# Two chained feed-forward layers behind a convolution: products that fill pauses, three slots in another order, and steps of the start moved

## The reference

```
w   = softmax(weight, axis=-1)                      # 8 heads x 7 taps
att = causal convolution of x over 7 tokens, one set of taps per head    # (4, 4096, 192)
h1  = att.reshape(16384, 192) @ w_in1               # 192 -> 2048
y1  = (h1 * cos(h1)) @ w_out1                       # 2048 -> 192
h2  = y1 @ w_in2
out = (h2 * clip(h2 + 3, 0, 6) / 6) @ w_out2
```

## Time and profile before

| | |
|---|---|
| median of 3 runs | 2235.25 us |
| the profiled execution | 2235.39 us, its span 2233.6 us |
| PE, DVE, ACT, POOL busy | 100%, 82%, 78%, 68% of the span |
| TensorE clock granted, mean | 0.999 |

### The profile page before, as it was taken

The page is one execution under the profiler, slowest core; times in us unless marked ns, Lnnn a source line. Parts: engine busy times, 40 slices in busy tenths (PEclk is TensorE's granted clock), DMA queues, the critical chain, the costliest instruction groups (busy, mean ns, idle before and its releaser), DMA issues.

```text
span 2233.6 us, 56658 instructions
## 1 busy us (share of the span) xinstructions
PE 2224.0 (100%) x19491; PEld 2200.1 (98%) x19491; DVE 1823.6 (82%) x2505; ACT 1732.6 (78%) x2841; POOL 1514.7 (68%) x1071
## 2 busy tenths in 40 slices
PE   9999999999999999999999999999999999999999
PEld 6899999999999999999999999999999999999998
DVE  8978888888888888888888888888888888888754
ACT  7888777787777877778877788777787777877775
POOL 7976666666666666766666666666666666666665
PEclk9999999999999999999999999999999999999999
DMA  4200000000000000000000000000000000000001
GB/s 107 58 8 16 15 10 4 14 14 14 14 0 14 14 14 14 0 14 14 14 14 7 7 14 14 14 13 1 14 14 14 14 0 14 14 14 7 4 6 23
DMA packets 208636, 33.27 MB, mean 15 GB/s; under 512 B 203152, under 2 KB 207248, under 8 KB 208592
## 3 DMA queue, kind: packets, MB, share of 16 engines
q1 hardware_dynamic: 205424, 32.27, 8.2%
q10 hardware_dynamic: 3168, 0.39, 0.1%
HBM read 19.92 MB, written 12.58 MB: 15 GB/s over the span
## 4 chain that ended last, share of the span: by engine, by line
PE 98%; DVE 1%; ACT 0%; DMA 0%; SPq 0%; issue 0%; DVEq 0%
PE h_ps L475 47%; PE acc L482 31%; PE acc_tail L489 21%; DVE acc L1002 0%; DMA x_in<-in_x 0%; DVE gate L930 0%; ACT pre L754 0%; DVE pre L919 0%; DVE wtail_hi L1044 0%; ACT pre L744 0%; ACT g_hi L758 0%; SPq L433 0%; ACT in_hi L887 0%; DVE acc L1001 0%; DVE xT L967 0%
## 5 line engine op out<-in xcount | busy, mean ns | idle before, releaser
L1186 POOL TENSOR_TENSOR g_lo<-gate,g_hi 128x512 fp32r<-128x512 f32 x1024 | 1470.5, 1458 | 702.1 <-ACT g_hi L758 701.2
L482 PE MATMUL acc<-g_hi,wout 64*128 64x512 f32 x4096 | 1416.4, 386 | 0.0
L475 PE MATMUL h_ps<-in_hi,win_hi 64*128 64x512 f32 x2048 | 790.7, 387 | 1.7 <-ACT in_hi L887 1.3
L489 PE MATMUL acc_tail<-g_lo,wout 64*128 64x512 f32 x2048 | 791.0, 386 | 0.0
L475 PE MATMUL h_ps<-in_lo,win_hi 64*128 64x512 f32 x2048 | 790.9, 387 | 0.0
L489 PE MATMUL acc_tail<-g_hi,wout 64*128 64x512 f32 x2048 | 790.7, 386 | 0.0
L482 PE MATMUL acc<-g_lo,wout 64*128 64x512 f32 x2048 | 790.4, 386 | 0.0
L475 PE MATMUL h_ps<-in_hi,win_lo 64*128 64x512 f32 x2048 | 790.3, 387 | 0.0
L475 PE MATMUL h_ps<-in_tail,wtail_hi 64*128 64x512 f32 x2048 | 790.0, 387 | 0.3 <-DVE in_tail L1069 0.3
L482 PEld LDWEIGHTS acc<-g_hi,wout 64*128 64x128 f32 x4096 | 753.4, 184 | 2.7 <-issue 0.3
L758 ACT ACTIVATE g_hi<-gate 128x512 fp32r<-128x512 f32 x1024 | 624.1, 631 | 114.1 <-DVE gate L933 55.0
(11 more groups left out here) (121 smaller groups left out, 2371.7 us busy)
## 6 DMA issues: line engine op xcount, KB each, us to landing
out_dram<-o_blk SPq DMA_DIRECT2D x128, 64.0 KB, 1.8
x_in<-in_x SPq DMA_DIRECT2D x126, 64.0 KB, 2.2
blk_tail<-in_x SPq DMA_DIRECT2D x62, 64.0 KB, 2.2
out_dram<-blk_tail SPq DMA_DIRECT2D x62, 64.0 KB, 1.8
stage<-in_moe_w_out SPq DMA_DIRECT2D x7, 384.0 KB, 3.3
stage<-in_moe_w_in SPq DMA_DIRECT2D x3, 512.0 KB, 4.4
stage<-in_moe_w_in SPq DMA_DIRECT2D x6, 256.0 KB, 3.9
pre<-in_moe_w_in SPq DMA_DIRECT2D x2, 256.0 KB, 4.6
```

The lines of the kernel that those rows point to most:

```text
L475: return pe.matmul(chunk_of(h_ps, q, half), w, x, start=start, stop=stop)
L482: return pe.matmul(acc[pair][:, :], wout[layer][rows, 2 * q + half, cols], g[rows, :], start=start, stop=stop)
L489: return pe.matmul(acc_tail[pair][:, :], wout[layer][rows, 2 * q + half, P:2 * P], g[rows, :], start=start, stop=stop)
L1186: pool.tensor_tensor(chunk_of(g_lo, q, half), chunk_of(gate, q, half), chunk_of(g_hi, q, half).bitcast(F32), ALU.subtract).then_inc(glo_re ...
```

## The change

- PE gets five pairs of products (`bridge`) between `convolve_tails` and the first slot. Their result, written to `h_ps` of slot 1, is overwritten there.
- Slot 0's first five products are made in the order 0, 2, 3, 4, 1 (the one with `in_lo` last), and ACT and DVE split tile 0's tail ahead of its main columns.
- In slots 0 to 2 PE's UP products are placed otherwise: slot 1 completes its own at its end, and the two products of `convolve_second` stand at the ends of slots 1 and 2.
- ACT rounds weight piece 5 in slot 0 behind the cosines and rounds `g_hi` of slot 0 in slot 1; DVE rounds piece 7 in slot 2 instead of 1, and POOL makes its rest in slot 3 instead of 2. One step of tile 1's convolution moves from slot 2 to 3 and one from 3 to 4.
- The two diagonals for `convolve_second` are made by DVE, not by POOL.
- `KEEP_1` goes from 0 to 6 and `LOW_TAIL_1` from 2 to 7.

```diff
-        HIGH_BY_DVE = {0: {0: 6, 1: 7, 3: 8, 5: 9}, ...
+        HIGH_BY_DVE = {0: {0: 6, 2: 7, 3: 8, 5: 9}, ...
-        STEP_ORDER = [0, 2, 1, 3, 4]
+        STEP_ORDER, FIRST_ORDER = [0, 2, 1, 3, 4], [0, 2, 3, 4, 1]
-        CONV_FIRST = [2, 2, 3, 5, 6, 7, 7, 7, 7]
+        CONV_FIRST = [2, 2, 3, 4, 5, 7, 7, 7, 7]
-        KEEP_1, TWIN_1, TAIL_1, LOW_TAIL_1, HIGH_1, LOW_1 = 0, 1, 2, 2, 5, 6
+        KEEP_1, TWIN_1, TAIL_1, LOW_TAIL_1, HIGH_1, LOW_1 = 6, 1, 2, 7, 5, 6
...
             def rest_of_upper(i, ph, q):
 
-                if 0 < q <= LAG and i < 4:
+                if q in (1, LAG) and i < 4:
                     first_upper(5 + i, ph, q - 1, ph.base + q - 1)
-                if 0 < q <= SECOND_BY_PE and i == 4:
-                    convolve_second(q - 1)
...
+                if q == 1:
+                    for i in range(5, 9):
+                        first_upper(i, ph, q, ph.base + q)
+                if q > 0:
+                    convolve_second(q - 1)
...
+            def bridge(count):
+
+                w = win_hi[L1]
+                for _ in range(count):
+                    for rows, half in ((LOW, 0), (UP, 1)):
+                        pe.matmul(chunk_of(h_ps, 1, half), w[rows, 0:P], w[rows, 0:TOK], start=True, stop=True)
...
             convolve_tails()
+            pe.wait_ge(whi_done, 1)
+            bridge(BRIDGE_PAIRS)
             phase(first_phase())
...
+                    if ph.setup == 0 and q == 1:
+                        high_half(0, 0, 0)
...
-                    high_part(q, slot, ph.setup != 0 or q >= G_BUFS, 1 if ph.setup in (0, 1) else 2)
+                    if ph.setup == 0 and q == 0:
+                        weight_high(5)
+                    else:
+                        high_part(q, slot, ph.setup != 0 or q >= G_BUFS, 1 if ph.setup in (0, 1) else 2)
...
+            act.wait_ge(tails_convolved, 1)
+            split_tail(acc_tail[1][0:DT, :], L2)
             for half in range(2):
...
-            act.wait_ge(tails_convolved, 1)
-            split_tail(acc_tail[1][0:DT, :], L2)
-            act.wait_ge(hi_ready[L2], 2)
+            act.wait_ge(hi_ready[L2], 1)
             split_twin(in_tail[L2][0:DT, :].bitcast(F32), L2)
-            for n in (4, 5):
-                weight_high(n)
+            weight_high(4)
...
+            dve.wait_ge(eye_step, 3)
+            for t in range(SECOND_BY_PE):
+                dve.tensor_scalar(diagonal_main(t), eye, taps[:, MAIN, t:t + 1], None,
+                                  ALU.mult).then_inc(main_diag_ready, 1)
...
-            pool.wait_ge(taps_ready, QUADS)
-            for t in range(SECOND_BY_PE):
-                pool.tensor_scalar(diagonal_main(t), eye, taps[:, MAIN, t:t + 1], None, ALU.mult).then_inc(diag_ready, 1)
```

More of the change, by code:

```diff
@@ L18 @@
 WARM_PAIRS = 9
+BRIDGE_PAIRS = 5
 G_BUFS = 4
@@ L201, in conv_moe_kernel @@
         diag_ready = sem("diag_ready")
+        main_diag_ready = sem("main_diag_ready")
         twin_copied = sem("twin_copied")
@@ L276, in conv_moe_kernel @@
         OUT_PIECES = {0: [4, 7, 8, 9], 2: [14, 15, 16, 17]}
-        HIGH_BY_DVE = {0: {0: 6, 1: 7, 3: 8, 5: 9}, 1: {0: 10, 1: 11, 2: 12, 4: 13, 7: 14}}
+        HIGH_BY_DVE = {0: {0: 6, 2: 7, 3: 8, 5: 9}, 1: {0: 10, 1: 11, 2: 12, 4: 13, 7: 14}}
         HIGH_IN = {2: {0: 15, 2: 16, 4: 17}}
@@ L282, in conv_moe_kernel @@
         LOW_FIRST, LOW_GATE = 6, 5
-        LOW_IN = {1: 6, 2: 7, 4: 8, 6: 9, 8: 10, 10: 11, 12: 12, 14: 13, 16: 14, 18: 15, 20: 16, 22: 17}
+        LOW_IN = {1: 6, 3: 7, 4: 8, 6: 9, 8: 10, 10: 11, 12: 12, 14: 13, 16: 14, 18: 15, 20: 16, 22: 17}
         MAIN, TAIL = 0, 1
@@ L508, in split_waits @@
                     pe.wait_ge(whi_done, 1)
-                    pe.wait_ge(hi_ready[L2], 1)
+                    pe.wait_ge(first_half, 1)
+                    pe.wait_ge(hi_ready[L2], 2)
                 if n == 1:
-                    pe.wait_ge(lo_ready[L2], 1)
+                    pe.wait_ge(lo_ready[L2], 2)
                 if n == 2:
@@ L515, in split_waits @@
                     pe.wait_ge(whi_done, 2)
-                    pe.wait_ge(lo_ready[L2], 2)
+                    pe.wait_ge(lo_ready[L2], 1)
                 if n == 4:
@@ L530, in first_lower @@
             def first_lower(i, ph, q, slot):
-                half, n = (0, STEP_ORDER[i]) if i < 5 else (1, i - 5)
+                half, n = (0, (FIRST_ORDER if ph.setup == 0 and q == 0 else STEP_ORDER)[i]) if i < 5 else (1, i - 5)
                 if i == 0:
@@ L604, in convolve_second @@
             def convolve_second(t):
-                pe.wait_ge(diag_ready, TAPS + t)
+                pe.wait_ge(main_diag_ready, t + 1)
                 if t == 0:
@@ L1028, in split_low_first @@
             def split_low_first():
+                dve.wait_ge(hi_ready[L2], 1)
+                dve.tensor_tensor(in_tail[L2][DT:P, :], acc_tail[1][0:DT, :], in_tail[L2][0:DT, :].bitcast(F32),
+                                  ALU.subtract).then_inc(lo_ready[L2], 1)
                 for half in range(2):
                     cols = slice(half * HALF, (half + 1) * HALF)
-                    dve.wait_ge(hi_ready[L2] if half else first_half, 1)
+                    dve.wait_ge(hi_ready[L2] if half else first_half, 2 if half else 1)
                     i = dve.tensor_tensor(in_lo[L2][:, cols], first_bank(half)[:, cols], in_hi[L2][:, cols].bitcast(F32),
@@ L1035, in split_low_first @@
                 i.then_inc(lo_ready[L2], 1)
-                split_low_tail(acc_tail[1][0:DT, :], L2, 0)
             def weight_high(n):
```

## The result

| | before | changed |
|---|---|---|
| median of 11 runs | 2236.0 us | 2241.34 us |
| lowest and highest | 2234.97, 2236.48 | 2240.38, 2243.86 |
| the profiled execution, its span | 2235.39, 2233.6 | 2240.39, 2238.7 |

The ratio is 1.0027, with an interval from 1.0019 to 1.0035. The change makes the kernel some 5 us slower (5.0 in the profiled executions, 5.3 in the medians; the interval is 4.2 to 7.8). The whole interval but its lowest edge lies above 0.2%. I had forecast 2239.5 and put most of the chance (0.55) on "no difference that can be told". That was wrong. The time is inside the range (2237.2 to 2241.8), and above the likeliest case's own one (up to 2240.8).

A forecast was written before the change was run, and what follows sets the result against it. The prediction took PE, busy without a break at 4.31 us a slot, to bound the kernel. Its terms, -1.2 + 3.65 + 1.7 = +4.15 on 2235.39, gave 2239.5 us, range 2237.2 to 2241.8.

The forecast's parts named there:

- the likeliest case: Whole kernel: the forecast as summed, 2239.5 us, own range 2238.3 to 2240.8, chance 0.70.
- gained at slot 7: Start through slot 7: earlier gates and piece 7 ready at 35.05 gain 1.2 us, bounds 0 to 2.0.
- stall ahead of slot 8, net: PE before slot 8 waits for in_tail behind slot 7's gates: 3.8 + 0.1 - 0.28 = 3.65 us, bounds 3.2 to 4.0.
- clock: After the stall PE's clock falls for one stretch, costing 1.7 us, bounds 0 to 3.4.
- the upper bound that I had named: Clock after the stall: at most 3.4 us, for two slow stretches.
- Bridge, diagonals, UP order: Start: bridge fills the pause, price 0; diagonals hidden on DVE, price 0; UP products give slot 0's h at 15.8.
- The early fall: Clock at 0.51 from 15.4 to 18.9 us, 1.7 us of PE's time; forecast to vanish with the bridge.
- the rival of diagonals that wait for POOL: First fraction: DVE's diagonals queue behind POOL, 0.9 us later, time 2240.4; chance 0.04.
- Whatever moves slot 9 moves the end: From slot 9 on: PE keeps its own pace of 4.31 us a slot, so the end moves by the same amount.
- the edge between "same" and "slower": Whole time: under 0.2% (4.47 us, up to 2239.7) counts as no change; same 0.55, slower 0.43.

The follow-up runs named there:

- tail_early: The changed kernel with LOW_TAIL_1 put back from 7 to 2, so tile 1's in_tail is made in slot 2 again: 2235.71 us, ratio 1.0006.
- before_tail_late: The kernel before with one number changed, LOW_TAIL_1 from 2 to 7: 2240.48 us (8 runs), ratio 1.0025.
- tail_6: The changed kernel with DVE's in_tail step at slot 6 (LOW_TAIL_1 = 6) instead of 7: 2236.35 us, ratio 1.0007.
- filled_stall_2: The changed kernel with 17 pairs of unused products that PE makes while it waits ahead of slot 8: 2240.82 us, ratio 1.0023.
- no_bridge: The changed kernel with LOW_TAIL_1 = 2 and BRIDGE_PAIRS = 0 in place of 5: 2236.17 us, ratio 1.0008.
- after_best: The changed kernel with in_tail at slot 4, piece 7 back in its old places and the second tile's halo copy one slot earlier: 2235.07 us, ratio 1.0003.
- piece7_back: The changed kernel with LOW_TAIL_1 = 2 and piece 7 back in its old places (DVE slot 1, POOL ahead of slot 2): 2234.36 us, ratio 1.0002.
- halo_early: The changed kernel with LOW_TAIL_1 = 2 and the second tile's halo copies in slot 8 instead of 9: 2234.37 us, ratio 1.0000.
- before_tail_5_halo: The kernel before with in_tail at slot 5 instead of 2 and the second tile's halo copy one slot earlier: 2233.31 us, ratio 0.9994.
- before_tail_5: The kernel before with in_tail at slot 5 instead of 2 (LOW_TAIL_1 = 5): 2234.06 us, ratio 0.9996.

## Why the prediction was wrong

By its own terms, each read in the profiled executions (slot 9 moved by 5.05, the profiled time by 5.00). The median of the eleven runs lies 0.95 above the profiled execution, and no profile shows what those runs add:

| term | forecast | measured |
|---|---|---|
| gained at slot 7 | -1.20 | -0.53 |
| stall ahead of slot 8, net | +3.65 | +3.93 |
| clock | +1.70 | +1.66 |
| sum | +4.15 | +5.06 |

- **The gain at slot 7** is the step that failed: -1.20 forecast, -0.53 measured. I let POOL's row begin at 20.1 and gave it 14.65 of work and 0.3 of gaps. It began at 20.26 and had 15.37 of work: 2.56 for piece 5 (2.36 before), 7.93 for six `g_lo` (7.70 summed), 2.29 for piece 7 (2.01). The result was piece 7 at 35.86, 0.81 late, where the forecast had only 0.95 to gain by it. All of the added work lies beside casts of DVE, which I had priced at nothing for POOL. I had read from the earlier trace rows only what a cast loses when POOL is first (1.80 in place of 0.69); when the cast is first, POOL pays. Piece 5 starts 0.39 behind the cast at 19.87. The third of the four `g_lo` at 28.22 (1.62 long, the others 1.29 to 1.30) starts at 30.73, while the cast of piece 7 runs (29.57 to 31.19). The last part of piece 7 (1.04) starts 0.30 behind the cast of piece 8. tail_early has the same row of POOL, but there DVE still has `in_tail` in slot 2, the cast of piece 8 comes 0.81 later, and that part takes 0.73. All twelve profiles fall out so: with a cast running at its start piece 5 takes 2.55 to 2.57, without 2.36 to 2.40; the last part of piece 7 1.03 to 1.04 with (three profiles), 0.73 to 0.76 without (nine). Changed kernel, then tail_early:

```profile
34.52 0.75 DVE L1065 CAST wout<-stage 128x768 fp32r<-128x768 f32 x1
```

```profile
33.52 1.98 POOL L1222 TENSOR_TENSOR wout<-stage,wout 128x512 fp32r<-128x512 f32 x2
35.33 0.59 DVE L1065 CAST wout<-stage 128x768 fp32r<-128x768 f32 x1
```

  Piece 7 is ready at 35.50 there, and slot 7 comes at 44.35 and not 44.66. So 0.31 of the missing gain came with the moved step itself.
- **The stall**: 4.10 and 0.11 to start again, less the old 0.28, where I had 3.8 and 0.1. PE's UP row lagged its LOW row by a step after the wait in slot 5, so slot 7's last h product stood 0.23 ahead of PE's next step, where it stands 0.45 ahead in slot 8 of the kernel before. tail_early and before_tail_late show that the moved step makes the stall, and tail_6 that it does so because it stands behind slot 7's gates.
- **The clock**: one stretch, 1.66. In filled_stall_2 products in the pause take the fall away, so it hangs on the pause, as far as one profile can show. before_tail_late shows that 6.83 us of it are possible, the upper bound that I had named.
- **Bridge, diagonals, UP order**: as forecast. The diagonals took 0.94 for both at 14.60. The first stood 0.74 beside a POOL step that had begun at 14.52 and ended at 15.26, the second took 0.28 behind it. So the rival of diagonals that wait for POOL came about, by some 0.46, and cost nothing, as DVE then stood idle for 1.05 until the first fraction at 16.60. The early fall is gone in the changed kernel and there in no_bridge, with the doubt told at that run.
- **"Whatever moves slot 9 moves the end"** was true for this change and is not true in general, as slots 16 and 24 take 0.47 and 0.26 over the pace even in the kernel before. The delays of 5.05, 5.13 (before_tail_late) and 2.11 (tail_6) reached the last slot within 0.04, the smaller ones of after_best and no_bridge (1.32 and 0.57) within 0.16. Of the gains against the kernel before, those of piece7_back, halo_early and before_tail_5_halo (1.07, 1.07 and 2.54) arrived within 0.1, but tail_early lost 1.40 on the way and before_tail_5 1.33, most of it at slot 16, by the place of two small copies. Had the forecast rested on its early gain, it could have failed there.
- **The chances**: the sum stood 0.2 under the edge between "same" and "slower", and I put 0.40 of 0.70 on the near side of it. The two terms that were off both lay on the far side. With the right gain alone the sum is 2240.2, past that edge. The edge itself was too coarse as well: the measured interval reaches 0.08% to either side, so even the +4.15 of the sum (0.19%) would have been told from no change.

## What to carry to other kernels

When a step moves behind another on an in-order engine, ask what the step ahead of it waits for: `in_tail` cost some 0.6 us at slot 2 of the kernel before (slot 4 to 5), 0.65 at slot 6 and 4.5 to 5.1 us at slot 7, without the slow stretch behind it, because there it stood behind work that needs the products it holds up. A gain at the start reaches the end only if each later hand-over on another engine moves with it; look for the next wait (here slot 8, then slot 16) before adding it to the sum. Don't sum an engine's row from durations measured while its neighbour was the one to wait: when the neighbour comes first, the row pays.

## What the runs showed of the hardware

- A DVE copy of 128x6 or 64x6 took 0.16 us, or 1.26 to 1.33, and then a POOL instruction started within 0.1 us of it; why other copies that start as near stay short isn't shown. A cast of 128x768 took 0.56 or 1.60, by a start 0.2 us apart. It holds the other way too: up to 60 us, every POOL `g_lo` of 128x512 that began while a cast of DVE ran took 1.37 to 1.76, most of them 1.62; all others took 1.27 to 1.33. The Trainium skill, page "SBUF — State Buffer", section "SBUF: two separate sides", calls the shared port pair an exclusive lock that is held for the whole instruction, whoever starts first; these rows agree, and so does the first diagonal (0.74, the second 0.28):

```profile
14.60 0.94 DVE L1189 TENSOR_SCALAR in_f<-sum_tail,taps 128x128 f32<-128x128 f32 x2
```

```profile
14.52 0.74 POOL L1231 TENSOR_TENSOR wtail_lo<-pre,wtail_hi 64x256 fp32r<-64x256 f32 x1
```

- TensorE can begin at half pace for longer in one run than in another. In tail_6's profile the six convolution products took 5.03 us (0.85 apart at first), in the changed kernel's 2.81 (0.43 apart):

```profile
6.54 5.03 PE L727 MATMUL acc_tail<-xT_tail,oT 128*128 128x512 f32 x6 [0.36 <-ACT acc_tail L898]
```

```profile
6.54 2.81 PE L727 MATMUL acc_tail<-xT_tail,oT 128*128 128x512 f32 x6 [0.79 <-ACT acc_tail L898]
```

```profile
13.02 0.47 PE L475 MATMUL h_ps<-in_hi,win_hi 64*128 64x512 f32 x1 [1.10 <-ACT in_hi L887]
```

```profile
13.24 0.47 PE L475 MATMUL h_ps<-in_hi,win_hi 64*128 64x512 f32 x1 [1.30 <-ACT in_hi L887]
```

  The two that fell are those whose clock rose earlier (first record at 5.19 and 5.48, against 6.46 and 6.58). The pause of 3.7 had the fall in both profiles in which PE was idle for it.
